# Earlier keys, copies on ScalarE and a shorter row of waiting products in a chunked delta-rule kernel

## The chip, the cores and the metric

One core of a Trainium2 chip runs the whole program. The metric is the device time of one execution in microseconds, and the time of a kernel is the median of its runs. Matrix products run on TensorE (PE), elementwise work on VectorE (DVE), ScalarE (ACT) and GpSimd (POOL). SyncE (SP) does no arithmetic: it issues most of the transfers from the device memory.

## The reference, cut to what matters

```python
k_n = k / (norm(k) + 1e-6)                       # B=4, H=8, S=768, D=48
for t in range(S):                               # a 48x48 state for each of 32 (batch, head) pairs
    y[:, :, t] = q_t @ state
    state = state + beta_t * outer(k_t, v_t - k_t @ state)
x = y reshaped to [3072, 384]
x = ((x @ w1) * (x @ w2)) @ w3 @ w_out           # 384 -> 1024 -> 1024 -> 384
# then: logits = x @ phi (32 slots), softmax over the tokens and over the slots,
# 8 experts of two matrices each on 4 slots, and the slots mixed back into the tokens
```

## The kernel before, in words

The 768 steps of the recurrence are cut into chunks of C = 32 tokens. Four chunks (STEPS = 4) make one iteration, so there are six iterations (n = 0 to 5) and 24 steps (g = n * 4 + s). The 32 pairs of batch and head lie side by side in the 128 partitions and along the columns.

An iteration needs two kinds of preparation, which depend on its keys and queries alone. The first is the grams: `gram_products` multiplies each chunk's keys with its keys and its queries, 64 columns for each pair, into one bank of PSUM for each chunk. The left half of a bank (keys with keys) goes to `Gs`; the right half (keys with queries) goes to `PT`, where the part that looks ahead in time has to be masked out by a multiplication with `upper`. The second is a triangular solve, thirty elimination steps of two elementwise instructions each (`update`). For iteration 0 DVE does it (`solve_first`), for the others POOL does it (`prep`), after DVE has found the norms of the keys (`set_up`, `set_up_root`, `set_up_rest`). The solved matrices are scaled and transposed into `TM` by DVE (`scale`, `turn_back`).

Each step g then runs on PE as `key_query_state`, `solve_rows`, `state_step` and `y_step`, with copies on ACT between them (`z_out`, `y_out`) and `r_rows` and `state` on DVE. Between these, PE runs the up projection of the step before (`up`), and DVE multiplies its two halves (`ab_mul`). The order of the work on each engine is written out by hand, and engines wait for each other by semaphores.

What lies ahead of step 0, and what the change touches:

- SP issues its transfers in this order: half of the keys and queries of iteration 0, `beta`, `phi`, `wot`, the two halves of `w3t` (line 310), the keys and values of iteration 0 (`load_kv(0, 0)`, line 307), `w1` (line 327) and `w2` (line 328), and after a wait for the first `part_ps` products those of iteration 1 (`load_kv(1, 1)`). In the text "values" means the tensors of `load_kv`, and "keys" those of `kq_piece`, which hold keys and queries for the grams.
- ACT issues the eight pieces of iteration 1's keys (line 527), in the middle of its copies for the folded weights.
- PE starts with `FILLERS` = 48 small products, then makes the grams of iteration 0, then folds the weights `phi`, `w_out` and `w3` into `P_sb` (lines 1182 to 1200), then waits for iteration 1's keys and makes its grams. Then come the `AWAKE` products (line 1211): one product of 128x512 for each k in 15 to 29, each after the wait for elimination step k of `solve_first`. Their results are never read. Only then does `body` start, with `solve_rows` of step 0.
- DVE masks iteration 0's left halves (`first_keys`, line 645), solves, scales and transposes, then masks chunk 0 of `PT[0]` (`first_pt`), then the four banks of iteration 1 straight from PSUM (`mask_pt`), then the rest of `PT[0]`, then adds the state of step 0, and then runs `set_up(1)`.
- ACT copies iteration 0's right halves raw into `PT[0]` (line 508), and iteration 1's left halves into `Gs` (`gram_out`).

Of the kernel before, what the change touches and what calls it, by code (L numbers as in the profile page):

```python
# [19 lines left out]
ACT = mybir.ActivationFunctionType  # L20
AX = mybir.AxisListType.X

B, H, S, D = 4, 8, 768, 48
C = 32
# [7 lines left out]


DOWN_LAG = 2
FILLERS = 48

AWAKE = range(15, 30)
ROOT_LINKS, ROOT_SPLIT = 14, 8

ROOT_SCALE, ROOT_MIN = 2.0 ** 64 / 1.457, 1e-19  # L40
# [57 lines left out]
def delta_moe_kernel(nc, kq, kv, beta, w1, w2, w3, w3t, wo, wot, phi, e1, e2, out):  # L98
    ctx = ExitStack()
    with ctx:  # L100
# [203 lines left out]
        @block.sync  # L304
        def _(sp):
            def load_kv(n, p):
                sp.dma_start(KV[p].rearrange("p a b c d -> p (a b c d)"), kv[n]).then_inc(kv_in[p], 16)

            def load_w3t(i):
                sp.dma_start(w3t_raw[i], w3t.rearrange("(c p) f -> p c f", p=128)[:, :, i * HF:(i + 1) * HF])\  # L310
                  .then_inc(w3t_in[i], 16)

            def reload_kq(n, p):

                for q in range(H // 2):
                    for r in range(2):
                        sp.dma_start(*kq_piece(n, p, q, r)).then_inc(kq_in[p][r], 16)

            for i in range(H // 2):
                sp.dma_start(*kq_piece(0, 0, i, 0)).then_inc(kq_first[i], 16)  # L320
            sp.dma_start(beta_sb[:], beta).then_inc(beta_in, 16)
            sp.dma_start(phi_sb[:], phi.rearrange("(c p) f -> p c f", p=128)).then_inc(phi_in, 16)
            sp.dma_start(wot_raw, wot.rearrange("(c p) f -> p c f", p=128)).then_inc(wot_in, 16)
            load_w3t(0)
            load_w3t(1)
            load_kv(0, 0)
            sp.dma_start(w_raw[0], w1.rearrange("(c p) f -> p c f", p=128)).then_inc(w12_in[0], 16)
            sp.dma_start(w_raw[1], w2.rearrange("(c p) f -> p c f", p=128)).then_inc(w12_in[1], 16)
            sp.wait_ge(part_ps, 2)
            load_kv(1, 1)  # L330

            def reload_kv(n, p):

                for s in range(STEPS):
                    sp.dma_start(KV[p][:, :, s].rearrange("p a h d -> p a (h d)"),
                                 kv[n].rearrange("p (a s f) -> p s a f", a=2, s=STEPS)[:, s]).then_inc(kv_in[p], 16)

            def reload(n, p):

                sp.wait_ge(qs_done, n * STEPS + STEPS - 1)  # L340
                reload_kq(n + 2, p)
                sp.wait_ge(kz_done, n * STEPS + STEPS)
                reload_kv(n + 2, p)

            for n in range(NIT - 2):
                reload(n, n % 2)

            sp.wait_ge(y_ps, (NIT - 1) * STEPS)
            sp.dma_start(w3_late, w3.rearrange("(c p) f -> p c f", p=128)).then_inc(w3_in, 16)

            sp.wait_ge(m_ps, 2 * (NIT - 1))
            for c in range(KC):
                sp.dma_start(w1_chunk(0, c), e1[0, c * 128:(c + 1) * 128]).then_inc(e1_in[0], 16)

            def load_e1(e):
                sp.dma_start(room1[e].rearrange("p (c f) -> p c f", c=KC),
                             e1[e].rearrange("(c p) f -> p c f", p=128)).then_inc(e1_in[e], 16)


            sp.wait_ge(tm_done, NIT)  # L360
            load_e1(1)

            sp.wait_ge(y_ps, NT)
            sp.dma_start(wo_late, wo.rearrange("(c p) f -> p c f", p=128)).then_inc(wo_in, 16)
            load_e1(2)

            sp.wait_ge(a_ps, 2 * NT)
            for e in (4, 6):
                load_e1(e)
            sp.wait_ge(ab_ps, 2 * NT)  # L370
            for e in (5, 7):
                load_e1(e)

            sp.wait_ge(m_ps, 2 * NIT)
            load_e1(3)
            for i, e in enumerate(E_ORDER):
                if i >= 2:
                    sp.wait_ge(h1_ps, i)
                sp.dma_start(room2(i).rearrange("p (c f) -> p c f", c=FC),
                             e2[e].rearrange("(c p) f -> p c f", p=128)).then_inc(e2_in[e], 16)  # L380
            out_v = out.rearrange("(b n w j) e -> n w b (j e)", b=B, n=NIT, j=STEPS)
            for n in range(NIT):
                sp.wait_ge(o_sb[0], 2 * n + 2)
                sp.wait_ge(o_sb[1], 2 * n + 2)
                sp.dma_start(out_v[n], OUT[n].rearrange("p j e -> p (j e)")).then_inc(out_done[n], 16)
            for n in range(NIT):
                sp.wait_ge(out_done[n], 16)
# [61 lines left out]
        def _(act):  # L449
# [52 lines left out]

            for i in range(H // 2):
                act.dma_start(*kq_piece(0, 0, i, 1)).then_inc(kq_first[i], 16)

            for s in range(STEPS):
                act.wait_ge(gs_done, s + 1)
                nc.scalar.activation(PT[0][:, s], first_gram[0][s][:].rearrange("p (h i) -> p h i", h=H)[:, :, C:2 * C],
                                     ACT.Copy).then_inc(pt_raw, 1)

            def w_high(i):
                act.wait_ge(w12_in[i], 16)
# [8 lines left out]
            part_out(1, 32 * KC)  # L521
            act.wait_ge(wp_ps, 1)
            nc.scalar.activation(wp_sb[:].rearrange("p a b -> p (a b)"), pK[:, 0:FC * NS], ACT.Copy).then_inc(wp_done, 1)

            for i in range(H // 2):
                for r in range(2):
                    act.dma_start(*kq_piece(1, 1, i, r)).then_inc(kq_in[1][r], 16)
            part_out(2, 128)
            part_out(3, 128)
            act.wait_ge(p_ps, 1)  # L530
            nc.scalar.activation(P_sb[:].rearrange("p a b -> p (a b)"), pY[:, 0:FC * NS], ACT.Copy).then_inc(p_done, 1)
            for s in range(STEPS):
                gram_out(1, s, first_gram[1][s])
            w_high(0)

            def body(n, p, k):
# [68 lines left out]
        def _(dve):  # L605
# [28 lines left out]

            def mask_pt(n, p, s, bank):

                dve.wait_ge(gs_done if n == 1 else gram_done, n * STEPS + s + 1)
                nc.vector.tensor_tensor(PT[p][:, s], bank[:].rearrange("p (h i) -> p h i", h=H)[:, :, C:2 * C],
                                        upper[:].unsqueeze(1).broadcast_to([128, H, C]),
                                        ALU.mult).then_inc(pt_mask, 1)  # L640
# [5 lines left out]
                                        bank[:].rearrange("p (h i) -> p h i", h=H)[:, :, 0:C],  # L646
                                        upto[:].unsqueeze(1).broadcast_to([128, H, C]), ALU.mult).then_inc(gs_done, 1)

            def first_pt(s0, s1):

                dve.wait_ge(pt_raw, s1)
                m = PT[0][:, s0:s1].rearrange("p s h i -> p (s h) i")
                nc.vector.tensor_tensor(m, m, upper[:].unsqueeze(1).broadcast_to([128, (s1 - s0) * H, C]),
                                        ALU.mult).then_inc(pt_mask, s1 - s0)

# [173 lines left out]
            def body(n, p, k):  # L829
                q = 1 - p  # L830
                for s in range(STEPS):
# [2 lines left out]
                    tp = q if s == 0 else p  # L834
                    fin, prep = not is_first(n), not is_last(n)
                    if g == 0:
                        first_pt(0, 1)
                        for i in range(STEPS):
                            mask_pt(1, q, i, first_gram[1][i])
                        first_pt(1, STEPS)  # L840
                        state(g)
                        set_up(1, q, k)
                        continue

                    def mask_at(i):
# [6 lines left out]
                    if g == 1:  # L852
                        set_up_root(1)
                        set_up_rest(1, q, k)
                    if g == 2:
                        w_low(1, 0)
                        w_low(1, 1)
                    if s == 1 and fin:
# [110 lines left out]
        def _(pe):  # L969
# [81 lines left out]
            def y_step(g, p, s):  # L1051

                pe.wait_ge(z_done, g + 1)
                if g < STEPS:
                    pe.wait_ge(pt_mask, 1 if g == 0 else 2 * STEPS)
                apart(pe, pe_passed)
                for h in range(H):
                    for b in range(B):
                        q, o = slice(32 * b, 32 * b + 32), 32 * (b ^ 1)
                        last = mm(pY[o:o + 32, h * D:h * D + D], PT[p][q, s, h, :], Z[q, h, :],  # L1060
                                  start=(g == 0 and h == 0), stop=(h == H - 1), skip_group_check=True)
                last.then_inc(y_ps, 1)

            def x_turn(t):
                pe.wait_ge(y_done, t + 1)
                if t > 0:
                    pe.wait_ge(abt_done, t * 2 - 1)
                else:
                    pe.wait_ge(pt_mask, 2)
                for c in range(KC):  # L1070
                    last = nc.tensor.transpose(pT[:, c * 128:(c + 1) * 128], xs[:, c * 128:(c + 1) * 128], ident[:])
                last.then_inc(xt_ps, 1)

            def up(t, half, w, sums=None, k0=0, k1=3 * KC):
# [3 lines left out]
                if t == 0:  # L1078
                    pe.wait_ge(xhi_done, 1)
                    pe.wait_ge(w12_in[w], 16)  # L1080
                    if half == 0:
                        pe.wait_ge(pt_mask, 3 + w)
                    else:
                        pe.wait_ge((a_done, ab_done)[w], 1)
                    for c in range(KC):
# [122 lines left out]
                gram_products(1, s, first_gram[1][s])  # L1208
            for k_ in AWAKE:
                pe.wait_ge(prep_link, X_LINK + 2 * k_)  # L1210
                mm(pK[:], ident[:], Macc[:, 0:HF], start=True, stop=True)  # L1211
            pe.wait_ge(p_done, 1)

# [204 lines left out]
```

## Time and profile before

| | us |
|---|---|
| median of 3 runs (lowest, highest) | 556.9 (555.53, 558.25) |
| the profiled execution's own time | 556.01 |
| its span, first to last instruction | 554.3 |
| PE busy | 491.6 (89%) |
| DVE busy | 244.5 (44%) |
| POOL busy | 184.1 (33%) |
| ACT busy | 139.9 (25%) |

The span is shorter than the execution's own time because the latter also holds what lies before the first and after the last instruction. A busy share is a mean over parts of the program with different limits: what a change in one part is worth has to be read in that part. Times in the rows are microseconds from the start of the span.

### The profile page before, as it was taken

How to read it: one execution, taken by the hardware profiler on the slowest of the kernel's cores; microseconds unless marked ns; L12 is line 12 of the kernel's file. 1: busy time of each engine (PE TensorE's matmuls, PEld its weight loads, DVE VectorE, ACT ScalarE, POOL GpSimd, SP SyncE). 2: the span in 40 equal slices, each digit the busy share in tenths (PEclk: the TensorE clock that was granted, in tenths of full speed). 3: DMA queues.
4: the chain of work that ended last, by engine and by line, in shares of the span. 5: the costliest groups of instructions: out<-in, count | busy, mean ns of one | idle time of the engine just before them, and what ended most of it. 6: DMA issues, size and time to landing. Idle time of an engine off the chain costs nothing.

```text
span 554.3 us, 24402 instructions
## 1 busy us (share of the span) xinstructions
PE 491.6 (89%) x11308; PEld 353.1 (64%) x11308; DVE 244.5 (44%) x539; ACT 139.9 (25%) x273; POOL 184.1 (33%) x334
## 2 busy tenths in 40 slices
PE   6733999987999989999999999899999999779974
PEld 5313556765777767777777777677777777334433
DVE  3796168324734426344283342733423321344424
ACT  1210232221232222222222222222222222203313
POOL 1001008881088600787018850288400000000000
PEclk9975999995999989999999999999999999789997
DMA  8996000170000620005300071000070416996948
GB/s 221 397 297 199 2 4 2 34 199 3 5 2 4 152 81 4 4 4 133 102 4 4 4 172 62 4 4 2 10 299 4 161 72 228 372 391 214 352 153 341
DMA packets 28437, 65.15 MB, mean 118 GB/s; under 512 B 1968, under 2 KB 15408, under 8 KB 28080
## 3 DMA queue, kind: packets, MB, share of 16 engines
q1 hardware_dynamic: 26992, 61.23, 33.2%
q10 hardware_dynamic: 1344, 2.36, 1.6%
q8 instruction: 89, 1.46, 1.1%
q14 instruction: 12, 0.10, 0.1%
HBM read 58.87 MB, written 4.72 MB: 115 GB/s over the span
## 4 chain that ended last, share of the span: by engine, by line
PE 76%; DMA 7%; POOL 7%; DVE 3%; issue 3%; ACT 1%; ACTq 1%; SPq 1%; DVEq 0%; POOLq 0%
PE pB L1105 17%; PE pA L1105 16%; DMA arena<-kq_dram 4%; POOL prep_slab L436 4%; PE pD L1047 3%; PE pK L1029 3%; PE pY L1060 3%; POOL prod_p L435 3%; PE pK L1007 3%; PE pK L1211 2%; PE pT L1121 2%; PE pG L1121 2%; PE pD L1129 2%; DMA arena<-wot_dram 2%; PE pY L1014 2%
## 5 line engine op out<-in xcount | busy, mean ns | idle before, releaser
L632 DVE TENSOR_TENSOR arena<-a_sb,pB 128x512 f32<-128x512 f32 x42 | 28.9, 687 | 139.5 <-PE pB L1105 139.3
L435 POOL TENSOR_TENSOR prod_p<-prep_slab 128x30 f32<-128x30 f32 (+9 forms) x150 | 74.5, 497 | 41.8 <-DVE prep_slab L698 30.9
L436 POOL TENSOR_TENSOR prep_slab<-prep_slab,prod_p 128x30 f32<-128x30 f32 (+9 forms) x150 | 81.6, 544 | 11.8
L1105 PE MATMUL pB<-whi,xhi 128*128 128x512 f32 x138 | 59.8, 433 | 0.0
L1105 PE MATMUL pB<-whi,xlo 128*128 128x512 f32 x138 | 54.6, 395 | 0.0
L1105 PE MATMUL pB<-wlo,xhi 128*128 128x512 f32 x138 | 54.4, 394 | 0.0
L1105 PE MATMUL pA<-whi,xlo 128*128 128x512 f32 x138 | 49.3, 407 | 3.5 <-DVE xlo L627 3.5
L1105 PE MATMUL pA<-whi,xhi 128*128 128x512 f32 x138 | 52.0, 432 | 0.0
L1105 PE MATMUL pA<-wlo,xhi 128*128 128x512 f32 x138 | 47.9, 401 | 0.0
L475 ACT ACTIVATE a_sb<-pA 128x512 f32<-128x512 f32 x48 | 28.8, 600 | 61.1 <-PE pA L1105 60.8
L428 POOL TENSOR_SCALAR_AFFINE_SELECT prep_slab<-prep_slab 128x1024 f32<-128x1024 f32 x5 | 6.3, 1264 | 112.5 <-DVE sys_s L666 112.5
L1014 PE MATMUL pY<-ST,arena 48*32 48x48 f32 x1472 | 32.1, 213 | 3.8 <-issue 3.8
L416 POOL TENSOR_TENSOR arena<-arena,nrm 128x1152 f32<-128x1152 f32 (+1 forms) x11 | 17.9, 1629 | 46.1 <-DVE prep_slab L720 45.3
L1105 PEld LDWEIGHTS pA<-whi,xlo 128*128 128x128 f32 x138 | 25.9, 190 | 11.4 <-DVE xlo L627 5.2
L1007 PE MATMUL pK<-ST,arena 48*32 48x48 f32 x1472 | 31.0, 212 | 1.3 <-issue 1.3
L623 DVE TENSOR_TENSOR ST<-pD,ST 112x768 f32<-112x768 f32 x24 | 23.0, 958 | 20.7 <-PE pD L1047 18.3
L989 PE MATMUL pT<-arena 48*32 48x64 f32 x640 | 14.8, 246 | 18.9 <-DMA arena<-kq_dram 16.5
L479 ACT ACTIVATE arena<-pT 128x512 f32<-128x512 f32 x24 | 14.4, 600 | 67.2 <-PE pT L1121 67.2
L1007 PEld LDWEIGHTS pK<-ST,arena 48*32 48x32 f32 x1472 | 27.3, 105 | 6.0 <-issue 6.0
L1105 PEld LDWEIGHTS pB<-whi,xhi 128*128 128x128 f32 x138 | 25.9, 188 | 7.1
L1105 PEld LDWEIGHTS pA<-wlo,xhi 128*128 128x128 f32 x138 | 26.7, 193 | 5.6
L1105 PEld LDWEIGHTS pB<-whi,xlo 128*128 128x128 f32 x138 | 25.9, 188 | 6.2
(246 smaller groups left out, 849.6 us busy)
## 6 DMA issues: line engine op xcount, KB each, us to landing
late_w<-e_dram SPq DMA_DIRECT2D x8, 1536.0 KB, 9.0
arena<-e_dram SPq DMA_DIRECT2D x5, 1536.0 KB, 10.4
arena<-kq_dram SPq DMA_DIRECT2D x36, 192.0 KB, 5.6
arena<-kv_dram SPq DMA_DIRECT2D x16, 384.0 KB, 5.9
out_dram<-late_w SPq DMA_DIRECT2D x6, 768.0 KB, 4.9
arena<-w3t_dram SPq DMA_DIRECT2D x2, 2048.0 KB, 19.2
arena<-w_dram SPq DMA_DIRECT2D x1, 4096.0 KB, 14.2
arena<-kv_dram SPq DMA_DIRECT2D x2, 1536.0 KB, 26.8
```

Source lines behind the costliest of these rows:

```text
L416: nc.gpsimd.tensor_tensor(v, v, nr, ALU.mult).then_inc(vp_done, 1)
L435: link(nc.gpsimd.tensor_tensor(pv, a, x, ALU.mult))
L436: link(nc.gpsimd.tensor_tensor(dst, dst, pv, ALU.add))
L475: nc.scalar.activation(a_sb[:], pA[:], ACT.Copy).then_inc(a_done, 1)
L623: nc.vector.tensor_tensor(ST[0:112], pD[0:112, :, 0:DM], ST[0:112], ALU.add).then_inc(s_done, 1)
L632: nc.vector.tensor_tensor(ab_tile(s, p)[:, half * HF:(half + 1) * HF], a_sb[:], pB[:], ALU.mult).then_inc(ab_done, 1)
L1007: last = mm(pK[32 * b:32 * b + 32, h * D:h * D + D], KQ[p][r:r + D, b // 2, h, 0, C * s:C * s + C], ST[r:r + D, b // 2, h * D:h * D + D], ...
L1014: last = mm(pY[o:o + 32, h * D:h * D + D], KQ[p][r:r + D, b // 2, h, 1, C * s:C * s + C], ST[r:r + D, b // 2, h * D:h * D + D], start=(h = ...
L1029: last = mm(pK[q, h * D:h * D + D], TM[p][q, s * H + h, :], R[q, h, :], start=True, stop=True)
L1047: last = mm(pD[r:r + D, b // 2, h * D:h * D + D], KV[p][q, 0, s, h, :], Z[q, h, :], start=True, stop=True)
L1105: last = mm((pA, pB)[w][:], lhs[:, c * 128:(c + 1) * 128], rhs[:, w, c, fc], start=(k == 0), stop=(k == 3 * KC - 1))
L1121: last = nc.tensor.transpose((pT, pG)[half][:, c * 128:(c + 1) * 128], ab_tile(s, p)[:, f0:f0 + 128], ident[:])
```

## The change

1. SP issues the eight pieces of iteration 1's keys right after the second half of `w3t`, ahead of the values of iteration 0 and of `w1` and `w2`. ACT issues them no more.
2. ACT copies both halves of iteration 1's grams, `gram_out(1, s)` and then `pt_copy(1, s)`. DVE no longer reads these banks.
3. On DVE, after `first_pt(0, 0, 1)` comes `set_up(1)`, then the state of step 0, then the mask for chunks 1 to 3 of iteration 0. All four chunks of iteration 1 are masked in one instruction at step 2, ahead of `w_low(1, 0)`. The waits of `y_step`, `x_turn` and `up` are adapted.
4. `FILLERS` is 47 instead of 48.
5. The waiting products: nine of 384 columns, after elimination steps 21 to 29, and three of 512 columns, one after the first residual (`r_done`) and two after `x_link`.

```diff
-FILLERS = 48
-AWAKE = range(15, 30)
+FILLERS = 47
+AWAKE = range(21, 30)
@@ SP
             load_w3t(1)
+            reload_kq(1, 1)
             load_kv(0, 0)
@@ ACT
-            for i in range(H // 2):
-                for r in range(2):
-                    act.dma_start(*kq_piece(1, 1, i, r)).then_inc(kq_in[1][r], 16)
...
+            def pt_copy(n, s):
+                nc.scalar.activation(PT[n][:, s], first_gram[n][s][:].rearrange("p (h i) -> p h i", h=H)[:, :, C:2 * C],
+                                     ACT.Copy).then_inc(pt_raw, 1)
             for s in range(STEPS):
                 gram_out(1, s, first_gram[1][s])
+                pt_copy(1, s)
             w_high(0)
@@ DVE
                     if g == 0:
-                        first_pt(0, 1)
-                        for i in range(STEPS):
-                            mask_pt(1, q, i, first_gram[1][i])
-                        first_pt(1, STEPS)
+                        first_pt(0, 0, 1)
+                        set_up(1, q, k)
                         state(g)
-                        set_up(1, q, k)
+                        first_pt(0, 1, STEPS)
                         continue
...
                     if g == 2:
+                        first_pt(1, 0, STEPS)
                         w_low(1, 0)
@@ PE, y_step / x_turn / up
-                if g < STEPS:
-                    pe.wait_ge(pt_mask, 1 if g == 0 else 2 * STEPS)
+                if g < 2 * STEPS:
+                    pe.wait_ge(pt_mask, 1 if g == 0 else (g // STEPS + 1) * STEPS)
...
-                    pe.wait_ge(pt_mask, 2)
+                    pe.wait_ge(gs_done, STEPS + 1)
+                    pe.wait_ge(pt_raw, STEPS + 1)
...
-                        pe.wait_ge(pt_mask, 3 + w)
+                        pe.wait_ge(gs_done, STEPS + 2 + w)
+                        pe.wait_ge(pt_raw, STEPS + 2 + w)
@@ PE, ahead of body
             for k_ in AWAKE:
                 pe.wait_ge(prep_link, X_LINK + 2 * k_)
+                mm(pK[:, 0:DM], ident[:], Macc[:, 0:DM], start=True, stop=True)
+            for sem_, i in ((r_done, 1), (x_link, 1), (x_link, 1)):
+                pe.wait_ge(sem_, i)
                 mm(pK[:], ident[:], Macc[:, 0:HF], start=True, stop=True)
```

## Rows read from the trace of the kernel before

**Rows 1.** The page: busy time by engine (share, instructions), and the instruction queue (packets, MB, share).
```profile
PE 491.6 (89%) x11308; PEld 353.1 (64%) x11308; DVE 244.5 (44%) x539; ACT 139.9 (25%) x273; POOL 184.1 (33%) x334
...
q8 instruction: 89, 1.46, 1.1%
```

**Rows 2.** The chain of waits in order of time, 0 to 130: start, length, what.
```profile
30.68 20.03 DMA arena<-kq_dram
...
56.96 13.07 PE pK L1211 x30
70.03 0.86 PE pK L1029 x64
...
82.03 1.24 DVE prep_slab L698
...
124.23 1.24 DVE prep_slab L717
```

**Rows 3.** The timeline of PE: start, length, instructions (two records a product), idle before.
```profile
13.53 0.64 PE L989 MATMUL pT<-arena 48*32 48x64 f32 x15
16.29 0.31 PE L989 MATMUL pT<-arena 48*32 48x64 f32 x1 [2.11 <-issue]
...
32.48 1.97 PE L1177 MATMUL pY<-same,TM 128*128 128x32 f32 x16 [1.89 <-ACT TM L517]
...
138.79 1.10 PE L989 MATMUL pT<-arena 48*32 48x64 f32 x64
```

**Rows 4.** The timeline of DVE.
```profile
13.93 0.60 DVE L645 TENSOR_TENSOR prep_slab<-pB,upto 128x256 f32<-128x256 f32 x1
16.64 0.59 DVE L645 TENSOR_TENSOR prep_slab<-pT,upto 128x256 f32<-128x256 f32 x1 [2.11 <-PE pT L989]
...
48.50 1.93 DVE L725 STREAM_TRANSPOSE TM<-prep_slab 128x1024 f32<-128x1024 f32 x1
...
58.00 0.95 DVE L653 TENSOR_TENSOR PT<-PT,upper 128x768 f32<-128x768 f32 x1
...
74.23 1.23 DVE L664 STREAM_TRANSPOSE prep_slab<-prep_slab 128x1024 f32<-128x1024 f32 x1
...
78.02 0.19 DVE L680 SCALAR_TENSOR_TENSOR sys_s<-sys_s 128x32 f32<-128x32 f32 x1
...
92.42 5.52 DVE L733 TENSOR_TENSOR wlo<-late_w,whi 128x512 fp32r<-128x512 f32 x6
```

**Rows 5.** The timeline of ACT: its transfer issues.
```profile
25.18 6.12 ACTq L527 DMA_DIRECT2D arena<-kq_dram  x8
```

**Rows 6.** The timeline of POOL: two of the elimination's instructions, side by side.
```profile
91.49 0.49 POOL L436 TENSOR_TENSOR prep_slab<-prep_slab,prod_p 128x150 f32<-128x150 f32 x1
...
92.64 0.84 POOL L436 TENSOR_TENSOR prep_slab<-prep_slab,prod_p 128x168 f32<-128x168 f32 x1
```

**Rows 7.** SP's issue of both w3t halves, then issue to landing for w3t, then values.
```profile
5.56 4.90 SPq L310 DMA_DIRECT2D arena<-w3t_dram  x2
...
DMA to landing us min/median/max: 16.9/19.2/21.6
...
DMA to landing us min/median/max: 22.4/26.8/31.2
```

**Rows 8.** Stretches: busy PE, PEld, DVE, ACT, POOL, granted PE clock, DMA share, GB/s.
```profile
22.00:24.00 2.00, 2.00 (x11) 2.00 (x11) 1.83 (x7) 0.00 (x0) 0.00 (x0) 1.00 1.05 386
34.00:36.00 2.00, 0.46 (x5) 0.34 (x4) 1.85 (x5) 0.38 (x1) 0.00 (x0) 0.80 1.05 292
...
56.00:58.00 2.00, 2.00 (x74) 1.43 (x63) 0.77 (x3) 1.60 (x3) 0.00 (x0) 1.00 0.03 8
...
110.00:116.00 6.00, 6.00 (x114) 4.58 (x102) 1.65 (x2) 1.21 (x3) 5.37 (x10) 1.00 1.01 211
```

**Rows 9.** Waits of PE, 80 to 560: total, times, longest.
```profile
PE pY L1014 <- issue: 3.8, 3, 2.2
PE pA L1105 <- DVE xlo L627: 3.5, 1, 3.5
```

More of the change, by code:

```diff
@@ L504, in _ @@
                 act.dma_start(*kq_piece(0, 0, i, 1)).then_inc(kq_first[i], 16)
+            def pt_copy(n, s):
+                nc.scalar.activation(PT[n][:, s], first_gram[n][s][:].rearrange("p (h i) -> p h i", h=H)[:, :, C:2 * C],
+                                     ACT.Copy).then_inc(pt_raw, 1)
             for s in range(STEPS):
                 act.wait_ge(gs_done, s + 1)
-                nc.scalar.activation(PT[0][:, s], first_gram[0][s][:].rearrange("p (h i) -> p h i", h=H)[:, :, C:2 * C],
-                                     ACT.Copy).then_inc(pt_raw, 1)
+                pt_copy(0, s)
             def w_high(i):
@@ L635, in mask_pt @@
             def mask_pt(n, p, s, bank):
-                dve.wait_ge(gs_done if n == 1 else gram_done, n * STEPS + s + 1)
+                dve.wait_ge(gram_done, n * STEPS + s + 1)
                 nc.vector.tensor_tensor(PT[p][:, s], bank[:].rearrange("p (h i) -> p h i", h=H)[:, :, C:2 * C],
@@ L647, in first_keys, with first_pt @@
                                         upto[:].unsqueeze(1).broadcast_to([128, H, C]), ALU.mult).then_inc(gs_done, 1)
-            def first_pt(s0, s1):
-                dve.wait_ge(pt_raw, s1)
-                m = PT[0][:, s0:s1].rearrange("p s h i -> p (s h) i")
+            def first_pt(n, s0, s1):
+                dve.wait_ge(pt_raw, n * STEPS + s1)
+                m = PT[n][:, s0:s1].rearrange("p s h i -> p (s h) i")
                 nc.vector.tensor_tensor(m, m, upper[:].unsqueeze(1).broadcast_to([128, (s1 - s0) * H, C]),
```

## The prediction

> **What bounds the kernel now.** I read the busy shares first: PE is busy for 89% of the span [rows 1], so a gain must come from a stretch in which PE waits or works for nothing. The chain of waits in order of time shows two such stretches ahead of step 0. For 20.03 us the chain is a transfer, the last of iteration 1's keys, landing at 50.7; then come iteration 1's grams until 56.96; then 13.07 us of L1211, the products whose result nobody reads; and only at 70.03 `solve_rows` of step 0 [rows 2]. Yet nothing in step 0 needs iteration 1's keys. What it needs is DVE's solve of iteration 0, whose last transpose ends at 48.50 + 1.93 = 50.43 [rows 4]. So 70.0 - 50.4 = 19.6 us pass between "step 0 could start" and "step 0 starts", because PE executes in order and the late grams and fifteen idle products stand ahead of it.
>
> Behind step 0 the chain runs through DVE's preparation of iteration 1 (L698 at 82.03), through POOL's elimination, and from 124.23 through scale and transpose to `xlo` [rows 2]; PE idles 3.5 us for that `xlo` [rows 9]. So the rest moves forward only as far as POOL's start moves forward, and that start hangs 12.0 us behind `solve_rows` of step 0 (70.03 to 82.03) through PE's step 0 and `key_query_state` of step 1. The quantity to predict is when `solve_rows` of step 0 starts. I call it T0; before it is 70.0.
>
> **Keys on SP's queue.** The second half of `w3t` is issued at about 6.2 and lands 21.6 us later, at 27.8 [rows 7]. Before, ACT issued the keys from 25.18 to 31.30 [rows 5], and they shared the DMA engines with 4.7 MB of values, `w1` and `w2` at 292 GB/s in all [rows 8]. Now they come alone behind `w3t`. Their 8 x 192 KB = 1.57 MB take 4.1 us at the 386 GB/s of the stretch in which `w3t` streams, and 7.5 us at the 211 GB/s of the stretch in which SP reloads just such pieces by themselves [rows 8]. The latter is the same shape on the same queue, so I take it: keys in place at 35.3. Bounds: 31.9, and about 40 if something of the sharing remains.
>
> What is queued behind them: the values of iteration 0 landed at 10.5 + 22.4 = 32.9 [rows 7] and now come 4 us after the keys, near 39.5; their reader, the first residual, stands at 46.5, just ahead of scale and transpose, so 5 us are left. `w1` and `w2` come near 44 and 48; the first product with `w1` is 4.4 us behind T0 and that with `w2` 8.4 us. All bytes together are those of before and ended near 53 with a slower mixture, so this edit costs nothing as long as T0 + 4 is later than 44. If the queue ran at the keys' 211 GB/s throughout, the values would be in at 42.8, still in time; `w2` at about 57.7 would be the first to be late, at T0 + 8.4 = 57.9 just not.
>
> ACT's 6.12 us of issuing go away. They held up two copies in the folding of the weights, whose last products start at 32.48 after a wait for ACT [rows 3, 5]; I estimate PE free for the grams at 33.3 instead of 34.5. The keys at 35.3 are later, so they decide.
>
> **Grams and waiting products.** PE's clock fell to the half level near 35, while PE did little [rows 8]. The grams took 56.96 - 50.95 = 6.0 us at that level; at the full level one bank takes 1.10 us, four 4.4 us [rows 3]. PE starts them nearly where the clock had fallen, so I expect most of them at the half level, the last ones not: 5.5 us, to 40.8. A product of 128x512 takes 13.07 / 15 = 0.87 us [rows 2], one of 384 columns by width 0.65. Nine of these are 5.9 us, to 46.7. Their waits are for elimination steps 21 to 29, which are over by 46.1 on DVE even without the next edit, so PE's own work is the later of the two. Three of 512 add 2.6 us, to 49.3, and with hand-overs T0 = 49.5 on PE's side.
>
> **FILLERS 47.** The grams of iteration 0 halt for 2.11 us with exactly one record left, by "issue", so for no semaphore [rows 3]; DVE's fourth left half starts at 16.64 instead of about 14.5 and the whole solve behind it is late by that [rows 4]. The instruction queue's 89 packets for 2 x 11308 PE instructions are one for every 254 [rows 1]: the halt looks like the boundary of such a packet, at a fixed count of instructions. One filler less (two records and their two weight loads) pulls the last record ahead of the boundary; the halt then falls into PE's wait for `wot`. DVE's side of T0 becomes 50.4 - 2.1 = 48.3. Nearest bound: nothing, if the halt isn't tied to the count. The Trainium skill (Runtime: NRT & Kernel Launch, "Instruction fetch mechanics") says that instructions come in blocks of 256 with the next block fetched ahead, a crossing being mostly hidden. By the word "hidden" this edit would be worth nothing; the row of 2.11 us says that under load it is not hidden. Since PE's side is the later one, either answer moves T0 by 1 us at most.
>
> So T0 is the later of 48.3 and 49.5: 49.5, a gain of 70.0 - 49.5 = 20.5 us.
>
> **DVE's new order.** Behind its transpose DVE masks chunk 0 (no longer than before), then runs `set_up(1)` (74.23 to 78.21, 4.0 us), then adds the state. The state is thus ready about T0 + 5.3; its reader, `key_query_state` of step 1, follows the first `w1` product at T0 + 7.2, so it is hidden with 2 us left. The mask of chunks 1 to 3 (0.95 us, L653) ends before the residual of step 1 at T0 + 8.5. The four masks straight from PSUM and ACT's four added copies (about 0.4 us each) lie ahead of T0 beside PE's waiting products. All of this counts nothing.
>
> At step 2 DVE gets a mask of 1024 elements: 0.95 x 4/3 = 1.3 us, ahead of `w_low(1, 0)`. It delays the following `ab_mul` and a transpose on PE by up to 1.3 us, inside the 3.5 us that PE later waits for POOL's chain [rows 9]. But it also runs beside POOL. POOL's steps lengthen from 0.49 to 0.84 us once DVE's `w_low` runs, at nearly the same size [rows 4, 6]. So 1.3 us more of DVE work of this kind costs POOL between 0 and 1.3 us; by the ratio 0.35/0.84, and because POOL's instruction may have to wait the whole mask out, I take 0.7. The Trainium skill (SBUF — State Buffer, "SBUF: two separate sides") says that a DVE instruction with two SBUF inputs shuts POOL out for its whole duration, and this mask has two where the four removed ones had one. By it the price would be the full 1.3 us and the sum 0.6 us later.
>
> **Sum.** 556.0 (the profiled execution) - 20.5 + 0.7 = 536.2. The median of before is 0.9 above that execution: 537.1.
>
> **Rivals.**
> (a) The halt stays, or another appears in iteration 1's grams. DVE alone would give T0 = 50.5, so 538.1. With one or two halts of 2.2 us in the grams, which now run under a full DMA load as those of iteration 0 did, T0 is 51.7 to 53.9, so 539.3 to 541.5. For it: halts by "issue" also stand elsewhere (3 before L1014, 3.8 us) [rows 9]. Against it: most packets come in time.
> (b) The keys come at the rate of the reading stream, 31.9: PE starts grams at 33.3 at the full level, its side is 46.8, DVE's 48.3 decides: T0 = 48.3, 535.9.
> (c) No gain: something else that `solve_rows` waits for lands late, the transfers behind the keys above all, and T0 stays near 70. The landings above speak against it; it would need `w1` 15 us later than its bytes say. 556.
> (d) The other side: fewer waiting products leave PE less busy, and the clock stays at the half level through steps 0 to 3. A bank of grams there costs 1.5 us against 1.1 [rows 2, 3]; products of 512 columns fill PE better and should come nearer to double. With 0.8 more, the 50 us of PE work between 70 and 120 grow by 40 us; the 20.5 gained and the 3.5 us that PE idles later cover 24, so the time would be 16 above before, 572. It decides once the half level lasts for more than some 30 us of busy PE. Against it: before, the clock was back at full level by 56, after 5 us of grams [rows 8].
>
> **How the numbers follow.** The forecast's mechanism with T0 within 1.2 us: 0.60; (a) 0.20; (b) 0.14; (c) 0.02; (d) 0.04. The unknown terms are the keys (-1.2 with (b), +4), halts in the grams (up to +4.4), POOL (-0.7 to +0.6), and the halts later in the program: all boundaries of instruction packets move by some 17 instructions against the work, and such halts, 3.8 us before L1014 alone [rows 9], can shrink or grow by 3. The range is 531.5 to 543. This kernel's measurement tells about 0.5% (2.8 us) from no change. Faster by more: 0.94; within: 0.02; slower: 0.04.
>
> **What would show it.** In the changed kernel's chain the transfer of keys and L1211 of 13 us are gone; `solve_rows` (L1029 before) starts near 49.5; iteration 1's grams begin near 35; the halt of 2.1 us stands behind the last gram of iteration 0; L698 of iteration 1 starts near 61.5; POOL's elimination takes within 1.3 us of its 41; the half-level stretch near 124 reappears 20 us earlier. I am wrong if T0 is above 54, if the values of iteration 0 or `w1` end a wait on the chain, or if POOL's chain no longer ends last and PE gives time back between steps 1 and 4.

## The result, and the profile after

The changed kernel takes 543.5 us (median of 4 runs, 541.53 to 550.33) against 556.5 for the kernel before in the same session: a ratio of 0.9751, 95% interval 0.9706 to 0.9797. It is 13.0 us faster by the medians, 13.9 by the ratio. The forecast was 537.1, 19.4 us faster, with a range of 531.5 to 543. Some executions of any kernel here take over a per cent longer at a lower granted clock; the ratios leave them out, and among those shown they are the changed kernel's run of 550.33 us and the profiled executions of e6 and e9 below. The median of all four runs lies 0.5 us above the range; that of the other three is 542.6, just inside it.

The profiled execution took 544.47 us. The page of the changed kernel, as [rows 1]:

```profile
span 542.7 us, 24391 instructions
...
PE 486.4 (90%) x11300; PEld 349.3 (64%) x11300; DVE 244.0 (45%) x536; ACT 140.9 (26%) x277; POOL 185.1 (34%) x334
...
q8 instruction: 89, 1.46, 1.1%
```

Its chain of waits in order of time, which answers to [rows 2]. L1214 and L1217 are the waiting products, L1030 is `solve_rows`, L700 is DVE's product that starts POOL's elimination, and L719 is the scaling behind it:

```profile
22.54 13.10 DMA arena<-kq_dram
35.64 0.25 issue
35.88 1.93 PE pT L990 x64
...
40.84 1.66 issue
...
43.82 7.70 PE pK L1214 x18
51.51 2.57 PE pK L1217 x6
54.09 0.86 PE pK L1030 x64
...
66.87 1.24 DVE prep_slab L700
...
110.01 1.24 DVE prep_slab L719
...
115.06 0.54 DVE xlo L629
```

The 20 us of transfer and the 13 us of L1211 have become 13 and 10, and T0, the start of `solve_rows` of step 0, came at 54.0 instead of 70.0. Down the chain the gain reads 15.9 at T0, 15.2 at L700 (82.03 in [rows 2]), 14.2 at the scaling (124.23) and 14.2 at `xlo` (129.28). At `solve_rows` of step 23 it is still 14.2, and at the end of the span 11.6.

The 0.8 us between T0 and L700 go in one halt. From T0 to that product the changed kernel needs 12.9 us, the kernel before 12.1. In between PE stops by "issue" in the middle of step 0's `state_step`:

```profile
57.52 0.66 PE L1048 MATMUL pD<-Z,arena 32*48 32x48 f32 x40 [0.62 <-issue]
```

Of the experiments below, e1, e11 and e12 have no halt there, and they need 12.0 to 12.1 us.

The last 2.6 us go in the tail of this one execution: TensorE's half level (the lower of its two clocks, a granted clock of 0.50 in the rows) lasted 13.7 us there (463.8 to 477.5) against 10.2 before, and the transfer of the last expert's weights took 10.13 us in the chain against 8.89. From step 23 to the end it took 103.9 us, against 101.2 before and 100.9 to 102.6 in the profiled executions of the twelve experiments, so I put this down to that execution and don't explain it further.

```profile
512.53 10.13 DMA late_w<-e_dram
```

PE's and then DVE's timeline of the changed kernel, as [rows 3] and [rows 4]:

```profile
14.02 0.65 PE L990 MATMUL pT<-arena 48*32 48x64 f32 x16
...
39.27 1.58 PE L990 MATMUL pB<-arena 48*32 48x64 f32 x50
42.50 0.36 PE L990 MATMUL pB<-arena 48*32 48x64 f32 x11 [1.66 <-issue]
```

```profile
14.85 0.59 DVE L647 TENSOR_TENSOR prep_slab<-pT,upto 128x256 f32<-128x256 f32 x1
...
46.71 1.99 DVE L727 STREAM_TRANSPOSE TM<-prep_slab 128x1024 f32<-128x1024 f32 x1
...
77.37 1.22 DVE L655 TENSOR_TENSOR PT<-PT,upper 128x1024 f32<-128x1024 f32 x1
```

The reader is to see three things. The halt with one record left is gone from the grams of iteration 0. A halt of the same kind now stands in iteration 1's grams, with 14 records of the third bank left. And DVE's transpose ends at 48.70, 5.3 us ahead of T0: PE was the later side by far. The stretches of PE's waiting products show why they took longer than by width (columns as in [rows 8]):

```profile
44.00:46.00 2.00, 2.00 (x4) 1.05 (x4) 1.86 (x6) 2.00 (x3) 0.00 (x0) 0.50 1.08 442
46.00:48.00 2.00, 2.00 (x5) 1.05 (x4) 1.93 (x3) 1.32 (x1) 1.19 (x1) 0.65 0.99 410
48.00:54.00 6.00, 6.00 (x17) 2.85 (x15) 4.89 (x10) 0.00 (x0) 2.20 (x2) 1.00 0.09 37
```

The clock, at full level again from 40.6, fell back to the half level at 44.0, behind the halt in the grams, and stayed there until 47.4. With 3.4 us of that level the nine products took 7.70 us instead of 5.9.

### The profile page after: what moved, and what is told of

Same layout as the page of the kernel before. It is cut to its first block, busy times and chain, and to the rows that moved or that the text cites. A ratio compares the mean times of both kernels' runs of the same rounds, so it can differ in the third digit from the quotient of the medians.

```text
span 542.7 us, 24391 instructions
## 1 busy us (share of the span) xinstructions
PE 486.4 (90%) x11300; PEld 349.3 (64%) x11300; DVE 244.0 (45%) x536; ACT 140.9 (26%) x277; POOL 185.1 (34%) x334
## 4 chain that ended last, share of the span: by engine, by line
PE 76%; POOL 7%; DMA 4%; SPq 4%; issue 4%; DVE 3%; ACT 1%; DVEq 0%; POOLq 0%
PE pB L1108 18%; PE pA L1108 16%; POOL prep_slab L437 4%; PE pD L1048 4%; PE pK L1030 3%; PE pY L1061 3%; POOL prod_p L436 3%; PE pK L1008 3%; DMA arena<-kq_dram 2%; PE pT L1124 2%; PE pG L1124 2%; PE pD L1132 2%; PE pY L1015 2%; SPq L317 2%; PE pT L990 2%
## 5 line engine op out<-in xcount | busy, mean ns | idle before, releaser
L1108 PEld LDWEIGHTS pB<-wlo,xhi 128*128 128x128 f32 x138 | 25.9, 188 | 4.3 <-issue 0.2
```

The source lines that it names most:

```text
L1108: last = mm((pA, pB)[w][:], lhs[:, c * 128:(c + 1) * 128], rhs[:, w, c, fc], start=(k == 0), stop=(k == 3 * KC - 1))
```

## The experiments

All landmarks in one table, from each kernel's profiled execution: T0, the starts of DVE's product, of the scaling and of `xlo` of step 4; "stretch" is the time from that `xlo` to `solve_rows` of step 23; then the median time and its ratio to the kernel before on the same chip.

| kernel | T0 | product | scaling | xlo | stretch | us | ratio (95%) |
|---|---|---|---|---|---|---|---|
| before | 70.0 | 82.0 | 124.2 | 129.3 | 323.8 | 556.5 | 1 |
| changed | 54.0 | 66.9 | 110.0 | 115.1 | 323.8 | 543.5 | 0.975 (0.971, 0.980) |
| e1 keys only | 58.5 | 70.6 | 113.0 | 118.0 | 321.9 | 543.6 | 0.979 (0.974, 0.984) |
| e2 keys on ACT | 64.4 | 76.9 | 120.1 | 125.1 | 321.4 | 552.1 | 0.993 (0.989, 0.997) |
| e3 no waiting products | 48.7 | 67.4 | 110.7 | 115.7 | 330.5 | 545.1 | 0.982 (0.977, 0.988) |
| e4 48 fillers | 54.0 | 67.0 | 110.1 | 115.2 | 323.2 | 542.9 | 0.977 (0.972, 0.983) |
| e5 mask at step 0 | 54.3 | 67.2 | 109.5 | 114.5 | 324.1 | 544.3 | 0.980 (0.970, 0.989) |
| e6 four of nine | 51.7 | 64.6 | 107.9 | 113.0 | 336.8 | 550.0 | 0.990 (0.985, 0.995) |
| e7 old masks | 56.0 | 69.2 | 111.6 | 116.7 | 325.7 | 543.8 | 0.979 (0.971, 0.987) |
| e8 loads later | 50.0 | 68.4 | 111.6 | 116.7 | 327.6 | 547.0 | 0.986 (0.979, 0.994) |
| e9 e6 + 5 small | 52.9 | 65.8 | 108.9 | 113.9 | 329.3 | 541.8 | 0.973 (0.968, 0.978) |
| e10 42 fillers | 53.5 | 66.7 | 110.0 | 115.0 | 334.6 | 552.9 | 0.989 (0.983, 0.996) |
| e11 e6 + 9 small + mask | 53.4 | 65.4 | 107.9 | 113.0 | 323.6 | 539.5 | 0.970 (0.965, 0.975) |
| e12 4 small | 55.8 | 67.8 | 111.0 | 116.1 | 323.8 | 541.5 | 0.975 (0.970, 0.980) |

The landmarks and the stretch are those of a single execution, which can lie some us off the median of its kernel: e6's took 554.1 us against a median of 550.0, e9's 545.9 against 541.8, e3's 549.1 against 545.1, and e2's 549.6 against 552.1. Each ratio is taken against the kernel before on the same chip in the same session.

**e1, the keys alone.**

```diff
 (the kernel before)
             load_w3t(1)
+            reload_kq(1, 1)
@@ ACT
-            for i in range(H // 2):
-                for r in range(2):
-                    act.dma_start(*kq_piece(1, 1, i, r)).then_inc(kq_in[1][r], 16)
```

> The kernel before with one edit: SP issues iteration 1's keys behind w3t, ACT issues none. Fifteen waiting products of 512 columns, 48 fillers and DVE's old order stay. Theory (the late keys alone held step 0 back, and PE's own work sets T0, the start of solve_rows of step 0): keys land near 35.5, grams end near 43.5, then 15 x 0.87 = 13.1 us of waiting products, so T0 = 57, some 13 us ahead of before (70.0), and a time of 544 to 546. Rival (DVE's old order, with its four masks straight from PSUM ahead of the state, costs much of the gain): T0 comes as said, but the start of L698's successor or POOL's chain moves less than T0, and the time is 549 or more.

Measured: keys at 35.18, T0 58.5, 543.6 us. That is about the theory's time (0.4 us below its range); T0 was expected at 57. The fifteen products took 14.6 us instead of 13.1, since the clock was at the half level from 43.6 to 47.0 here too. The keys no longer decided when the grams began: PE's own folding of the weights ended at 36.40. This one edit holds most of the change's gain: the ratios 0.979 and 0.975 can't be told apart. In the trace the rest of the change gives 4.5 us more at T0 and 2.9 at `xlo`.

**e2, the changed kernel with the keys on ACT's queue.**

```diff
-            reload_kq(1, 1)
@@ ACT, ahead of part_out(2, 128)
+            for i in range(H // 2):
+                for r in range(2):
+                    act.dma_start(*kq_piece(1, 1, i, r)).then_inc(kq_in[1][r], 16)
```

> The changed kernel with one edit undone: ACT issues iteration 1's keys again. Theory (PE's side sets T0, parts add up on it): keys land near 50.5, grams of 6 us to 56.7, then nine products of 384 columns (5.9) and three of 512 (2.6), T0 = 65.3, so 4.7 us ahead of before, a time of 551 to 553. Rival (the other parts are worth nothing without the keys): 556. Rival (they carry the gain): 546 or less.

Measured: T0 64.4 and 552.1 us, as the theory said. Its grams start at 50.39, when the transfers are over. They run through without a halt:

```profile
50.39 1.93 PE L992 MATMUL pT<-arena 48*32 48x64 f32 x64 [15.95 <-DMA arena<-kq_dram]
52.07 1.96 PE L992 MATMUL pA<-arena 48*32 48x64 f32 x64
53.78 1.17 PE L992 MATMUL pB<-arena 48*32 48x64 f32 x64
54.74 1.10 PE L992 MATMUL pG<-arena 48*32 48x64 f32 x64
```

From 50.39 to 55.84 that is 5.45 us, the 5.5 of the prediction, and the clock, at full level from 53.9, did not fall back behind them. The changed kernel needed 7.9 for the same grams.

**e3, no waiting products at all.**

```diff
-            for k_ in AWAKE:
-                pe.wait_ge(prep_link, X_LINK + 2 * k_)
-                mm(pK[:, 0:DM], ident[:], Macc[:, 0:DM], start=True, stop=True)
-            for sem_, i in ((r_done, 1), (x_link, 1), (x_link, 1)):
-                pe.wait_ge(sem_, i)
-                mm(pK[:], ident[:], Macc[:, 0:HF], start=True, stop=True)
```

> The changed kernel without all twelve waiting products (their results are read by nobody). Theory (PE was 5.4 us later than DVE, by products whose result nobody reads): T0 falls from 54.0 to DVE's 48.8, the time by 5 us to 538. Rival (d) of the prediction (the products hold TensorE's clock up): the half level lasts through steps 0 to 3, PE's work there grows by a third or more, and the time is 545 to 570.

Measured: T0 fell to 48.7 exactly as the theory said, and DVE's product came at 67.4, 0.5 us later than with the products; the time is no better. A part of its chain of waits, and a stretch of it:

```profile
48.70 1.21 PE pK L1030 x49
49.91 0.35 issue
...
51.49 1.50 PE pY L1061 x64
52.99 1.14 PE pD L1048 x48
54.13 1.03 issue
...
57.14 5.44 PE pA L1089 x6
```

```profile
58.00:62.00 4.00, 4.00 (x6) 1.35 (x4) 0.00 (x0) 1.74 (x1) 0.00 (x0) 0.50 0.01 4
```

PE idled from 45.3 to 48.7, and its clock stayed at the half level until 62.4. The first `w1` product took 5.44 us against 2.84, `y_step` 1.50 against 0.88, and two issue halts add 1.4. So step 0 began 5.3 us earlier and ended 0.5 us later. Rival (d)'s mechanism exists, but it lasted 17 us here, and together with the two halts it cost what T0 had gained. e3 also moves all that follows by 48 PE instructions against their old places, and its stretch is 6.7 us longer than the changed kernel's; what a shift alone can do is shown by e9 and e10 below, so e3's time can't be laid to the waiting products alone.

**e4, 48 fillers.**

```diff
-FILLERS = 47
+FILLERS = 48
```

> The changed kernel with 48 fillers instead of 47. Theory (the halt is bound to a count of PE instructions, and DVE isn't what sets T0): a halt of about 2 us with one record of iteration 0's grams left is back, DVE's transpose ends near 50.8 instead of 48.7, T0 stays at 54 and the time within 1 us of the changed kernel's. Rival (the halt depends on the load of the DMA engines alone): no halt at that place. Rival (DVE does set T0): T0 and the time 2 us later.

Measured: the halt is back at the same record, DVE's transpose ends at 50.29 instead of 48.70, T0 stays at 54.0, and the time (542.9) is that of the changed kernel. The halt is real, bound to the count, and worth nothing here.

```profile
13.26 0.65 PE L990 MATMUL pT<-arena 48*32 48x64 f32 x15
16.12 0.31 PE L990 MATMUL pT<-arena 48*32 48x64 f32 x1 [2.21 <-issue]
```

**e5, iteration 1's mask at step 0.**

```diff
                         first_pt(0, 1, STEPS)
+                        first_pt(1, 0, STEPS)
                         continue
...
                     if g == 2:
-                        first_pt(1, 0, STEPS)
```

> The changed kernel with the mask of iteration 1 (1024 elements, DVE) moved from step 2 to step 0, behind the mask of chunks 1 to 3, where DVE idles 3.2 us. Theory (that mask costs POOL's elimination its time, since both ran side by side): POOL's chain from DVE's product at 66.9 to the scaling at 110.0 shrinks from 43.1 to 42.3 us as before the change, the time falls by 0.8 us to about 542.7, and POOL's step at that place no longer stands out. Rival (the longer chain comes from something else, such as the instruction's own place in POOL's stream): 43.1 stays, the time 543.5.

Measured: POOL's chain took 42.3 us (67.17 to 109.47) instead of 43.1, as the theory said. The time, 544.3 us with an interval of 2% width, can't show 0.8 us. POOL's instruction that overlaps the mask in the changed kernel, and then the same one in e5, where only `w_low` follows:

```profile
77.49 1.48 POOL L437 TENSOR_TENSOR prep_slab<-prep_slab,prod_p 128x168 f32<-128x168 f32 x1
```

```profile
77.81 0.92 POOL L437 TENSOR_TENSOR prep_slab<-prep_slab,prod_p 128x168 f32<-128x168 f32 x1
```

**e6, four waiting products of 384 columns instead of nine.**

```diff
-AWAKE = range(21, 30)
+AWAKE = range(26, 30)
```

> The changed kernel with four instead of nine products of 384 columns; the three of 512 stay. Theory (PE has to be busy until DVE is ready, but no longer): grams end near 43.9, four products 3.3 us at a partly halved clock, three 2.6 us, T0 = 50 instead of 54.0, the clock back at the full level by 47.5 as before, iteration 1's product on DVE at 63 instead of 66.9, the time 539.5. Rival (without the long row the instructions of step 0 aren't there in time, as in the run without any waiting products): T0 = 50, but step 0 is interrupted by issue halts and the product stands at 65 or later, the time 542 to 544.

Measured: T0 at 51.7 and the product at 64.6, so 2.1 us gained at `xlo`, and yet 550.0 us: slower than the changed kernel by more than both intervals. Neither theory had this. The first 113 us had improved and the next 330 had got longer, although not one instruction was changed there. What had changed is their place: five products fewer, that is ten matmul records and their ten weight loads, 20 PE instructions, stand ahead of them. That led to e9, e10 and e12.

**e7, the part on ACT and DVE undone.**

```diff
 (the kernel before with e1's edits, and)
-FILLERS = 48
-AWAKE = range(15, 30)
+FILLERS = 47
+AWAKE = range(21, 30)
@@ PE: the twelve waiting products of the changed kernel
```

> The changed kernel with the part on ACT and DVE undone: DVE masks iteration 1 straight from PSUM ahead of the state, ACT copies only the left halves. Keys, 47 fillers and the twelve waiting products as in the changed kernel. Theory (that part hides no wait and costs POOL's chain): T0 = 54 as in the changed kernel, from there 12.1 us to DVE's product instead of 12.8, POOL's chain 42.3 instead of 43.1, so the scaling at 108.5 to 109.3 and the time 542 to 543. Rival (the part is what lets state and set_up be in time): the product comes 14 us or more behind T0, the time 545 or more.

Measured: POOL's chain 42.4 us as expected without the late mask. T0 came at 56.0 instead of 54, since the half level lasted until 49.5 in this execution; from T0 to the product 13.2 us, with an issue halt of 0.90. The time is 543.8. The part has no effect that can be measured; the 0.8 us of POOL it costs is the one thing that the runs (e5, e7) show of it.

**e8, the later loads held back until the grams are done.**

```diff
             load_kv(0, 0)
+            sp.wait_ge(gram_done, 2 * STEPS)
             sp.dma_start(w_raw[0], ...
```

> The changed kernel with SP waiting for the last gram of iteration 1 before it issues w1, w2 and the values of iteration 1. Theory (PE's halt in those grams comes from instruction transfers that stand behind data): the DMA engines are idle from about 40, the halt of 2 us near 40.5 is gone or shorter, the grams take 5.5 to 6.5 us instead of 7.9, T0 = 52 to 53, w1 lands near 47 and w2 near 51, both in time, the time 541.5 to 542.5. Rival (the halt is bound to the count of instructions alone): the halt stays 2 us, T0 = 54, the time 543.5.

Measured: the halt in the grams is gone (35.70 to 41.49, 5.8 us) and T0 is 50.0, better than expected. But the loads now run from 42 on, under step 0, and there the halt is, twice as long:

```profile
39.08 1.51 PE L991 MATMUL pB<-arena 48*32 48x64 f32 x64
...
52.39 0.48 PE L1049 MATMUL pD<-Z,arena 32*48 32x48 f32 x24
56.18 0.66 PE L1049 MATMUL pD<-Z,arena 32*48 32x48 f32 x40 [3.30 <-issue]
```

```profile
50.00:54.00 4.00, 2.17 (x153) 1.90 (x153) 2.00 (x5) 1.67 (x3) 1.05 (x1) 1.00 1.05 435
```

```profile
58.04 5.49 PE pA L1090 x6
```

Behind this halt the clock was at the half level from 57.0 to 63.9, and the first `w1` product took 5.49 us instead of 2.84. The product on DVE came at 68.4 and the time was 547.0. For this halt the cause is confirmed: without the load it is gone, and the load's new place has one. The expected time was missed, because the load has to be somewhere, and because a halt costs more than its own length when the clock falls behind it.

**e9, e10 and e12, the place alone.** e9 is e6 with five products of 32x32 behind the grams, e10 the changed kernel with 42 fillers, e12 the changed kernel with four such small products.

```diff
 e9: AWAKE = range(26, 30), and ahead of the waiting products (e12: range(4), AWAKE unchanged)
+            for k_ in range(5):
+                mm(pK[0:32, 0:32], ident[0:32, 0:32], ident[0:32, 0:32], start=True, stop=True)
 e10:
-FILLERS = 47
+FILLERS = 42
```

> The kernel with four waiting products of 384 columns, plus five products of 32x32 (some 0.1 us) behind iteration 1's grams, so that step 0 stands at the same PE instruction (1422 records before it) as in the changed kernel. Theory (the run with four products gained 2.1 us by xlo of step 4 and lost it later because all later instructions moved by 20 against the points at which PE halts for instructions): xlo near 113, steps 4 to 23 take the 324 us of the changed kernel instead of 337, the time 541 to 542. Rival (the four-product run lost its time through fewer waiting products, by the clock or otherwise): the time stays at 547 to 550.

> The changed kernel with 42 instead of 47 fillers (0.08 us less work at the start, nothing else), so that step 0 stands at 1402 PE records as in the run with four waiting products. Theory (the place of the instructions against the halts is worth several us by itself): T0 within 1 us of 54, but later halts at other work, steps 4 to 23 take 328 to 337 us instead of 324, the time 546 to 550. Rival (the place is worth nothing): 543.5.

Measured: e9 takes 541.8 us (ratio 0.973) where e6, which has five tiny products less, took 0.990. e10 takes 552.9 us (0.989) where the changed kernel took 0.975: less work, and slower by 1.4%. Both as the theory said, e10 even slower than it said, and in both pairs the intervals don't meet. PE's waits by "issue" from 130 to 455, in the changed kernel and then in e10:

```profile
PE pK L1008 <- issue: 2.4, 1, 2.4
PE pY L1015 <- issue: 2.1, 1, 2.1
PE pK L1030 <- issue: 2.0, 2, 1.1
PE pD L1048 <- issue: 1.9, 2, 1.3
```

```profile
PE pY L1015 <- issue: 7.4, 3, 3.5
PE pK L1008 <- issue: 2.6, 1, 2.6
PE pD L1048 <- issue: 2.2, 2, 1.3
PE pK L1030 <- issue: 1.3, 2, 0.9
```

The longest of e10's stands in the chain at 394.92, 3.8 us behind SP's issue of `w3` (391.09), 4 MB long. Behind it the clock fell, as the next stretch shows:

```profile
394.92 3.45 issue
```

```profile
398.50:401.80 3.30, 3.30 (x13) 2.70 (x12) 0.00 (x0) 0.60 (x1) 0.00 (x0) 0.50 1.03 422
```

The halts alone don't account for e10's stretch, 10.8 us longer than the changed kernel's. By the trace 4.4 us of it are idle time by "issue", and the other 6.4 are the same PE instructions taking longer. In e10 the half level came back three times, for 3.4 us each, at or just behind long halts (190.2, 258.5 and 398.4); in the changed kernel it stood nowhere between 123 and 463. In all, e10's stretch had 20.6 us of it, the changed kernel's 7.4. Across the halt at 394.92 e10 fell behind by 5.2 us, 3.45 of them the halt itself.

> The changed kernel with four products of 32x32 behind iteration 1's grams and nothing else, so that step 0 stands at 1438 PE records instead of 1422. Theory (the place alone is worth some us, and 1438 is a good one): T0 at 54 to 55, xlo of step 4 near 115.3, steps 4 to 23 in 322 to 324 us, the halts near 250 and 333 gone or short, the time 541.5 to 543. Rival (the best kernel's gain over the changed one came from the waiting products and the mask alone): steps 4 to 23 as in the changed kernel, the time 543.5 to 544.

Measured for e12: 541.5 us is in the expected range, but the stretch stayed at 323.8 and the ratio is the changed kernel's. The long halt near 250 shrank to 0.6, but a halt of 1.4 at 345 and 3.4 us at the half level (from 186.2) took its place, and T0 was 1.7 us later because the half level lasted until 49.7. The place of the kernel before is no better than the changed kernel's by anything that these runs can tell; the theory's second half, that this place is a good one, fell.

**e11, the sum of what helped**: e6's four products, nine small ones and e5's mask.

> The kernel with four waiting products of 384 columns, nine products of 32x32 behind iteration 1's grams (step 0 at 1438 PE records, as in the kernel before and in the keys-only run) and iteration 1's mask at step 0. Theory (halts and mask add up): xlo of step 4 near 112.2 (2.1 from the four products, 0.8 from the mask), steps 4 to 23 in 322 to 324 us as in those two kernels, the time 539 to 540.5, the fastest of all. Rival (place and waiting products don't add up this way): 543 or more.

Measured: 539.5 us, ratio 0.970 (0.965 to 0.975), in the expected range. By its trace `xlo` came at 113.0 rather than 112.2. Its interval overlaps the changed kernel's, so that it is faster than that one is likely, not shown.

```profile
65.45 1.24 DVE prep_slab L700
...
107.91 1.24 DVE prep_slab L719
```

## Why the prediction was right in kind, with a gain 6 us too large

- **The late keys held step 0 back, through PE's order.** Right. e1 and e2 show it from both sides.
- **Keys in place at 35.3** from the rate of the same pieces in a later stretch: 35.64. Right; with the faster row they would have been at 31.9. (Rival (b)'s PE side for that case adds up to 46.4 rather than 46.8; DVE's 48.3 decides either way.)
- **What is queued behind the keys costs nothing.** Right: no transfer of values, `w1` or `w2` ends a wait on the chain.
- **Grams 5.5 us.** This term failed: 7.9. Without DMA load they take 5.45 (e2) or 5.8 (e8). A halt of 1.7 us accounts for most of the difference; the rest goes with the clock, which came back 4.7 us into the grams here and 3.5 us into them in e2. The halt was in the text as rival (a), with a chance of one in five. It stood at the same place in PE's stream in all kernels whose grams ran under load.
- **Nine products of 384 columns in 5.9 us.** This term failed: 7.7. By width it is right (6.07 us in e8, at the full level), but in the changed kernel the clock fell back behind the halt. It did so in no kernel whose grams had no halt (e2, e8). The sum had the clock at full level from the end of the grams on.
- **T0 = 49.5.** It was 54.0, just at the bound above which the prediction calls itself wrong. The sum named the right side (PE, not DVE) and missed two terms on it, 2.4 and 1.8 us; the grams also began 0.6 us later, and 0.3 came back in the hand-over. That 54.0 meets the top end of rival (a), 53.9, is luck: there it stands for two halts, here it was one halt and a clock that fell back.
- **The gain at T0 passes down the chain.** Right but for the halt of step 0 (0.8 us), and only as long as PE stays busy up to T0. e3 shows the error of the idea that an earlier T0 is a gain by itself: 48.7 gave nothing.
- **FILLERS 47.** Right in the mechanism and in its being off the path (e4). The halt fell into the wait for `wot`. The Trainium skill (Runtime: NRT & Kernel Launch, "Instruction fetch mechanics") calls a block crossing mostly hidden. In the changed kernel six halts by "issue" were longer than 1 us, against 89 instruction packets; in e10 one was 3.45 us long.
- **DVE's order costs nothing, the late mask 0.7 on POOL.** Right: 0.8 to 0.9 (43.1 against 42.3 in e5). The Trainium skill's full exclusion (SBUF — State Buffer, "SBUF: two separate sides") gave 1.3, and POOL's chain lost less than the mask's 1.22. In kind the trace agrees: POOL's instruction starts 0.12 us behind the mask, ends 0.38 us behind the mask's end and takes 1.48 us. In e5 the same instruction takes 0.92 beside `w_low`, so a part of the price was paid without the mask too.
- **Halts later in the program move by 3 us at most.** In the changed kernel they left the stretch at 323.8, which was luck: a shift of some instructions either way gave 324 (e12) or 335 us (e10). The size was wrong, e10's extra being 10.8 us.

From the forecast's 536.2 for the profiled execution to the 544.5 that it took it is some 8 us: 4.6 at T0, 0.8 by the halt of step 0, 0.2 in POOL's chain and 2.6 in the tail of that one execution. Without the tail that is 5.6 us, and the median of 542.6 lies 5.5 above 537.1.

## What to carry to other kernels

When an engine executes in order, look for work that waits for a late transfer ahead of work that doesn't, and cost the path by what the engine does under the new conditions: the same grams took 5.45 us beside a quiet DMA and 7.9 beside a busy one. Idle products ahead of a critical step are not waste up to the moment when the step is ready: taking all of them away gained nothing (e3), taking away five of twelve gained 2.1 us at `xlo` (e6). And before a difference of 1% is put down to an edit, shift the instructions by some harmless ones and measure again: here five tiny products were worth 1.7% (e6 against e9) where the whole edit was worth 2.5%.

## What the runs showed of the hardware that was not expected

PE halts by "issue" at fixed places of its stream. Numbering PE's weight loads from the start (nearly each has one matmul record beside it), the halts of over 1.5 us stand at the same numbers whatever work lies there: 613, 3983 and 5798 in the changed kernel, 355, 613 and 3983 in e4, 227, 613, 3983, 5798 and 9556 in e10. The distances are multiples of about 129.6 loads, so of some 259 loads and matmul records. The page of the profile has 22,907 of these to 89 instruction packets, 257 to one. That the halts are waits for such packets is an inference from this agreement.

What decides whether a place halts PE stays open. For place 613 it was the load: it halts PE by 1.3 to 2.2 us in all eleven kernels whose grams of iteration 1 ran beside transfers, not in e2 or e8, and e8 halts at 871 instead, 258 loads later, where its load had gone. But load is not needed in general. Place 2168 or 2169 halts PE by 1.1 to 2.8 us in ten kernels with at most 20 GB/s under way. And at place 8131 of e9 PE stood for 1.58 us while nothing was transferred:

```profile
336.87 0.40 PE L1048 MATMUL pD<-Z,arena 32*48 32x48 f32 x4 [1.58 <-issue]
```

```profile
335.30:336.80 1.50, 0.00 (x0) 0.00 (x0) 0.00 (x0) 0.27 (x1) 0.00 (x0) 1.00 0.00 0
```

The longest halt was 3.6 us (e6, at place 9556, beside the transfer of `w3`).

TensorE's clock was at the half level just behind the halt in the grams in every kernel that had one: it fell back there, or in e6 and e7 had not yet risen. With waiting products it came back to the full level between 46.9 (e10) and 50.4 us (e11). I can name no difference in the work for that spread. It moves T0 by up to 2 us between kernels whose PE work ahead of it is nearly the same (54.0 in the changed kernel, 55.8 in e12, 56.0 in e7).
